# Up-projections of a feed-forward stage as seven products of quarters, on one core

## What is computed

```python
# x: 4608 x 512, w1, w2, w3: 512 x 768, w_out: 768 x 512, all float32
def _moe2_ref(x, w1, w2, w3, w_out):
    h = np.maximum(np.maximum(x @ w1, x @ w2), x @ w3)
    return (h @ w_out).astype(np.float32)
```

## Time and profile before

| | |
|---|---|
| median of 3 runs | 1120.35 us (1119.95 to 1121.66) |
| the profiled execution | 1120.02 us, its span 1118.2 us |
| mean granted clock of TensorE | 0.998 of full speed |
| first and second stage | 0 to 523.52 us |
| third stage | 523.52 to the end, nine blocks |
| bytes moved by DMA | 90.83 MB, mean 81 GB/s |

### The profile page before, as it was taken

The page is one execution under the profiler, slowest core; times in us unless marked ns, Lnnn a source line. Parts: engine busy times, 40 slices in busy tenths (PEclk is TensorE's granted clock), DMA queues, the critical chain, the costliest instruction groups (busy, mean ns, idle before and its releaser), DMA issues.

```text
span 1118.2 us, 14218 instructions
## 1 busy us (share of the span) xinstructions
PE 1099.5 (98%) x5938; PEld 890.4 (80%) x5938; DVE 464.0 (41%) x798; ACT 339.1 (30%) x555; POOL 144.9 (13%) x133
## 2 busy tenths in 40 slices
PE   7999999999999999999999999999999999999998
PEld 5776676888888888888888888888888888888887
DVE  3775677786568476551221302122131212212121
ACT  5566665334334324321121211212121121211211
POOL 0011453322033200237000000000000000000000
PEclk9999999999999999999999999999999999999999
DMA  9997852431231221113001020200102010010100
GB/s 261 324 263 234 233 196 105 137 115 39 78 116 57 97 78 38 57 50 127 32 24 52 1 76 1 76 1 20 57 1 76 1 60 16 19 58 1 38 1 38
DMA packets 65198, 90.83 MB, mean 81 GB/s; under 512 B 19696, under 2 KB 44272, under 8 KB 63472
## 3 DMA queue, kind: packets, MB, share of 16 engines
q1 hardware_dynamic: 61648, 73.81, 20.9%
q0 software_dynamic: 3488, 16.13, 4.1%
HBM read 61.21 MB, written 30.80 MB: 82 GB/s over the span
## 4 chain that ended last, share of the span: by engine, by line
PE 95%; ACT 3%; DMA 1%; DVE 1%; issue 0%; SPq 0%; ACTq 0%
PE ps L1033 39%; PE ps L587 27%; PE ps L1041 13%; PE ps L762 3%; PE ps L942 3%; PE ps L807 2%; PE ps L596 2%; PE ps L732 2%; DMA k_raw<-in_k_dram 1%; PE ps L691 1%; ACT packed L1155 1%; PE ps L786 1%; ACT ost L1307 1%; ACT a2T L1079 1%; PE ps L637 0%
## 5 line engine op out<-in xcount | busy, mean ns | idle before, releaser
L1033 PE MATMUL ps<-ys_lo,w_s_hi 128*128 128x512 f32 x648 | 252.1, 389 | 0.0
L1033 PE MATMUL ps<-ys_hi,w_s_hi 128*128 128x512 f32 x648 | 252.1, 389 | 0.0
L1033 PE MATMUL ps<-ys_hi,w_s_lo 128*128 128x512 f32 x648 | 252.1, 389 | 0.0
L1579 DVE TENSOR_TENSOR second<-ps,first 128x512 f32<-128x512 f32 x54 | 37.4, 692 | 305.7 <-PE ps L1033 305.7
L1033 PEld LDWEIGHTS ps<-ys_lo,w_s_hi 128*128 128x128 f32 x648 | 121.6, 188 | 25.3
L1033 PEld LDWEIGHTS ps<-ys_hi,w_s_hi 128*128 128x128 f32 x648 | 121.6, 188 | 25.3
L1033 PEld LDWEIGHTS ps<-ys_hi,w_s_lo 128*128 128x128 f32 x648 | 121.6, 188 | 25.2
L1079 ACT ACTIVATE h_hi<-third 128x512 fp32r<-128x512 f32 x54 | 34.1, 632 | 304.7 <-DVE third L1583 304.7
L587 PE MATMUL ps<-ln_hi,w_out_s_lo 128*128 128x512 f32 x280 | 109.0, 389 | 0.0
L587 PE MATMUL ps<-ln_lo,w_out_s_hi 128*128 128x512 f32 x280 | 108.9, 389 | 0.0
L587 PE MATMUL ps<-ln_hi,w_out_s_hi 128*128 128x512 f32 x280 | 108.9, 389 | 0.0
(11 more groups left out here) (140 smaller groups left out, 1411.4 us busy)
## 6 DMA issues: line engine op xcount, KB each, us to landing
y_features<-yst SPq DMA_DIRECT2D x9, 1024.0 KB, 4.5
y_raw<-y_features SPq DMA_DIRECT2D x9, 1024.0 KB, 5.4
out_dram<-ost SPq DMA_DIRECT2D x36, 256.0 KB, 2.1
k_raw<-in_k_dram SPq DMA_DIRECT2D x32, 256.0 KB, 5.9
v_raw<-in_v_dram SPq DMA_DIRECT2D x8, 1024.0 KB, 6.8
q_raw<-in_q_dram SPq DMA_DIRECT2D x32, 256.0 KB, 5.3
m_merged<-merged POOLq DMA_DIRECT2D x5, 1024.0 KB, 5.1
weight_raw<-in_moe_w_dram POOLq DMA_DIRECT2D x9, 512.0 KB, 4.3
```

The source lines that it names most:

```text
L1033: last = pe.matmul(ps[:, 3 * (c % 2) + w, :], w_max3[w][a][:, kk, c * P:(c + 1) * P], ys[z][:, kk, :], start=(kk == 0 and e == 0), stop=(k ...
L1579: dve.tensor_tensor(tmp2[c % 2][:, :], ps[:, 3 * (c % 2) + 1, :], tmp1[c % 2][:, :], ALU.max)\
```

## The change

For four pairs of blocks (1024 tokens each) the three up-projections are made as seven products of quarters in place of eight (Strassen's scheme in Winograd's form). The weight is cut in halves of its 512 inputs and, for an index i of 0 to 2, in the chunks i and i + 3 of its outputs; y is cut in halves of its features and in its two blocks. A group (`GROUPS` = 9 in a pair) is one i and one of w1, w2, w3. Its seven products go into four banks, three of them on top of what stands there (`PRODUCTS`: weight operand, y operand, bank). ScalarE copies the first product (`copy_first`) and the third (`copy_fifth`), VectorE adds up the quarters of the result, C11 in the bank itself, C21, C22 and C12 in SBUF (`spot` tiles), and keeps the maxima over w1, w2, w3 in four `best` tiles. In the third group of an i, ScalarE's `hi_h2` and VectorE's `low` split the four. The ninth block is computed as before, in groups of two banks (`plain_group`).

The operands of y are seven, three of them copies and four sums (T1 to T4), made by `hi_y` and `lo_y` in two halves of a pair. Those of the weights (S1 to S4 among them) are made and split by GpSimd in the second stage (`split_operands`, nine sets), stored in DRAM (`w_operands`) and streamed back by SyncE, one load of 128 x 3584 values for each group, in a ring of three buffers (`load_slot`). The output projection runs over a pair at once, eight tiles in eight banks. SBUF is laid out anew, and `y_raw` takes half of a pair at a time. Stages one and two are otherwise as before.

```diff
+GROUPS = 3 * MH
+RING = 3
+A21, A22, A11, A12, S1, S2, S3, S4 = range(8)
+B11, B21, B22, T1, T2, T3, T4 = range(7)
+PRODUCTS = ((A11, B11, 0), (S2, T2, 1), (S1, T1, 2), (A22, T4, 3), (A12, B21, 0), (S3, T3, 1), (S4, B22, 2))
...
+    w_dram = nc.dram_tensor("w_operands", (GROUPS, P, 8, 2, KH, P), F32).ap()
...
+            def load_slot(g):
+                t, s = divmod(g, GROUPS)
+                if g >= RING:
...
+                    sp.wait_ge(g_filled, group_end(g - RING))
...
+                    dst, src = slots[g % RING][:, :, :, :, :], w_dram[s][:, 1:8]
...
+                             src.rearrange("p o e k n -> p (o e k n)")).then_inc(slot_loaded[g % RING], 16)
...
+                for s in range(GROUPS):
+                    load_slot(GROUPS * t + s + RING)
+                for j in range(TPF):
+                    store_out(TPF * t + j)
+                    if j == 1 and t < FOUR - 1:
+                        sp.wait_ge(y_split, 2 * Y_PARTS * (t + 1) + Y_PARTS)
+                        load_y(t + 1, 1)
...
+            def split_operands(s):
+                n = W2_END + s
...
+                add(0, 0, raw[:, A21], raw[:, A22], ALU.add, 4 * s)
+                add(1, 2, raw[:, A11], raw[:, A21], ALU.subtract, 0)
+                add(2, 1, sums[:, 0, :, :], raw[:, A11], ALU.subtract, 4 * s + 1)
+                add(3, 3, raw[:, A12], sums[:, 1, :, :], ALU.subtract, 4 * s + 3)
...
+                pool.tensor_scalar(stage[:, 0:4, 0, :, :], raw, 1.0, None, ALU.mult).then_inc(weight_hi, 1)
+                pool.wait_ge(weight_hi, n + 1)
+                pool.tensor_tensor(stage[:, 0:4, 1, :, :], raw, stage[:, 0:4, 0, :, :].bitcast(F32), ALU.subtract)\
+                    .then_inc(weight_split, 1)
+                wait_alone(pool, weight_split, n + 1)
+                pool.dma_start(w_dram[s][:, 0:4], stage[:, 0:4, :, :, :].bitcast(F32)).then_inc(w_stored[0], 16)
...
...
+                pool.tensor_scalar(stage[:, 4:8, 0, :, :], sums[:, :, :, :], 1.0, None, ALU.mult).then_inc(sums_hi, 1)
+                pool.wait_ge(sums_hi, s + 1)
+                pool.tensor_tensor(stage[:, 4:8, 1, :, :], sums[:, :, :, :], stage[:, 4:8, 0, :, :].bitcast(F32),
+                                   ALU.subtract).then_inc(sums_split, 1)
+                pool.wait_ge(sums_split, s + 1)
+                pool.dma_start(w_dram[s][:, 4:8], stage[:, 4:8, :, :, :].bitcast(F32)).then_inc(w_stored[1], 16)
...
             for t in range(1, BLOCKS):
-                if t == BLOCKS - 1:
-                    wait_alone(pool, h_filled, 32)
-                    split_piece(W1_END)
                 block_scale(t)
-                if t < W1_END:
-                    split_piece(t)
-            split_pieces(W1_END + 1, W1_END + 3)
-            wait_alone(pool, h_filled, TPB * BLOCKS)
-            split_pieces(W1_END + 3, len(pieces))
+                for _ in range((0, 1, 2, 1, 1, 2, 1, 1, 0)[t]):
+                    split_operands(s)
+                    s += 1
...
+            def group(g):
...
+                pe.wait_ge(slot_loaded[g % RING], 16 * (g // RING + 1))
...
+                for n, (a, b, k) in enumerate(PRODUCTS):
+                    if n == 4:
+                        pe.wait_ge(first_copied, g + 1)
+                    elif n == 5:
+                        pe.wait_ge(second_ready, g + 1)
+                    elif n == 6:
+                        pe.wait_ge(fifth_copied, g + 1)
+                    if s == 0 and n in (0, 1, 2, 3, 5):
+                        pe.wait_ge(y_split, 2 * Y_PARTS * t + Y_PARTS + (1, 2, 3, 5, 0, 6)[n])
+                    for kk in range(KH):
+                        for e, (i, j) in enumerate(PASSES):
+                            last = pe.matmul(ps[:, group_bank(g, k), :], w[:, a - 1, i, kk, :], ys[:, b, j, kk, :],
+                                             start=n < 4 and kk == 0 and e == 0,
+                                             stop=kk == KH - 1 and e == len(PASSES) - 1, skip_group_check=n >= 4)
+                    last.then_inc(g_filled, 1)
...
+            def outputs(t, tiles):
...
+                down2(TPF * t, early)
+                down2(TPF * t + 1, early)
+                pe.wait_ge(h2_split, base + parts * (MH - 1) + 2)
+                down2(TPF * t, late)
+                down2(TPF * t + 1, late)
...
+            for t in range(FOUR):
+                for s in range(GROUPS):
+                    group(GROUPS * t + s)
+                outputs(t, TPF)
...
+            def hi_y(t, kk):
...
+                copy(ys[:, B11:B21 + 1, 0, kk, :], y_raw[:, :, 0, :]).then_inc(y_hi, 1)
+                act.wait_ge(turn_ready, 4 * half + 2)
+                copy(ys[:, T2, 0, kk, :], turn[1][:, :]).then_inc(y_hi, 1)
+                copy(ys[:, T1, 0, kk, :], turn[0][:, :]).then_inc(y_hi, 1)
+                copy(ys[:, B22, 0, kk, :], y_raw[:, 1, 1, :]).then_inc(y_hi, 1)
+                act.wait_ge(turn_ready, 4 * half + 3)
+                copy(ys[:, T4, 0, kk, :], turn[1][:, :]).then_inc(y_hi, 1)
+                act.wait_ge(turn_ready, 4 * half + 4)
+                copy(ys[:, T3, 0, kk, :], turn[0][:, :]).then_inc(y_hi, 1)
...
+            def copy_first(g):
+                act.wait_ge(g_filled, FILLS * g + 1)
+                if g >= 2:
+                    act.wait_ge(third_ready, g - 1)
+                copy(firsts[g % 2][:, :], ps[:, group_bank(g, 0), :]).then_inc(first_copied, 1)
...
+            def hi_h2(g):
...
+                for ready, m, c in ((best11, 0, 0), (best21, 1, 0), (best22, 1, 1), (best12, 0, 1)):
+                    act.wait_ge(ready, best_count(g))
+                    copy(h2[0][:, MH * m + i, c * BLK:(c + 1) * BLK], best[m][c][:, :]).then_inc(h2_hi, 1)
...
+                    copy_first(g)
+                    copy_fifth(g)
+                    if s % 3 == 0:
+                        copy_best(g)
+                    elif s % 3 == 2:
+                        hi_h2(g)
+                if t < FOUR - 1:
+                    hi_y(t + 1, 0)
+                else:
+                    hi_last_y()
+                for j in range(2):
+                    copy_out(TPF * t + j)
+                if t < FOUR - 1:
+                    hi_y(t + 1, 1)
+                for j in range(2, TPF):
+                    copy_out(TPF * t + j)
...
+            def lo_y(t, kk):
...
+                dve.tensor_tensor(turn[0][:, :], b12, b11, ALU.subtract).then_inc(turn_ready, 1)
+                dve.wait_ge(turn_ready, turns + 1)
+                dve.tensor_tensor(turn[1][:, :], b22, turn[0][:, :], ALU.subtract).then_inc(turn_ready, 1)
+                dve.wait_ge(y_hi, his + 1)
+                lo(ys[:, B11:B21 + 1, 1, kk, :], y_raw[:, :, 0, :], ys[:, B11:B21 + 1, 0, kk, :]).then_inc(y_split, 1)
...
+                low(4, B22, b22)
+                dve.wait_ge(y_split, his + 2)
+                dve.tensor_tensor(turn[1][:, :], turn[1][:, :], b21, ALU.subtract).then_inc(turn_ready, 1)
+                dve.wait_ge(y_split, his + 3)
+                dve.tensor_tensor(turn[0][:, :], b22, b12, ALU.subtract).then_inc(turn_ready, 1)
+                dve.wait_ge(turn_ready, turns + 4)
+                low(5, T4, turn[1][:, :])
+                low(6, T3, turn[0][:, :])
...
+            def group(g):
...
+                dve.wait_ge(first_copied, g + 1)
+                dve.wait_ge(g_filled, FILLS * g + 2)
+                wait(dve, c12_ready, g)
+                add(second_sum, bank[1], firsts[g % 2][:, :], second_ready)
+                if w > 0:
...
+                    keep(0, 0, bank[0], best11)
+                dve.wait_ge(g_filled, FILLS * g + 6)
+                wait(dve, c22_ready, g)
+                add(third_sum, bank[1], firsts[g % 2][:, :], third_ready)
+                dve.wait_ge(third_ready, g + 1)
+                dve.wait_ge(fifth_copied, g + 1)
...
+                c21, c22, c12 = (part[0], part[1], part[0]) if w else (best[1][0], best[1][1], best[0][1])
+                add(c21, third_sum[:, :], bank[3], c21_ready, ALU.subtract)
+                add(c22, third_sum[:, :], fifths[g % 2][:, :], c22_ready)
+                if w == 2:
...
+                    low(1, 0, 0)
+                if w > 0:
+                    dve.wait_ge(c21_ready, g + 1)
+                    if w == 2:
+                        dve.wait_ge(best21, best_count(g) - 1)
+                    keep(1, 0, c21[:, :], best21)
+                    dve.wait_ge(c22_ready, g + 1)
+                    if w == 2:
+                        dve.wait_ge(best22, best_count(g) - 1)
+                    keep(1, 1, c22[:, :], best22)
+                dve.wait_ge(second_ready, g + 1)
+                dve.wait_ge(g_filled, FILLS * g + 7)
+                if w > 0:
+                    dve.wait_ge(best21, best_count(g))
+                add(c12, bank[2], second_sum[:, :], c12_ready)
+                if w == 2:
+                    low(2, 1, 0)
+                if w > 0:
+                    dve.wait_ge(c12_ready, g + 1)
```

(6 more changed lines are left out.)

535 lines of the change are left out of this document (347 added, 188 removed).

## The result

The changed kernel takes **1072.55 us** (median of 4 runs, 1071.46 to 1072.93). The kernel before took 1121.01 us beside it (4 runs, 1119.95 to 1123.04). The ratio is 0.9564, 95% interval 0.9548 to 0.9581, so the change saves 4.4%, or 48.5 us. The forecast was 1073.0 us. The profiled execution after has a span of 1071.0 us against 1118.2: 47.2 us less.

A forecast was written before the change was run, and what follows sets the result against it. TensorE, busy for 98% of the span, was taken as the limit. 1120.0 - 49.0 - 3.5 + 4.0 + 1.3 = 1072.8 us, with 0.3 for the median 1073 us; range 1067 to 1090 us.

The forecast's parts named there:

- Removed matmuls: Third stage: four pairs of blocks save 216 up-projection matmuls at 0.2267 us each, -49.0 us.
- Output tiles' wait: Output projection: with a bank per tile, the third tile's 0.39 us wait for ScalarE's copy goes nine times, -3.5 us.
- nine blocks are alike: Third stage of the old kernel: each of nine blocks was taken to have the same 0.39 us idle.
- Boundaries: After third groups inside a pair TensorE waits for ScalarE's copy, 0.5 us at 8 boundaries: +4 us, bounds 0 to 16.
- GpSimd in the second stage: GpSimd's added work makes VectorE wait at shared SBUF interfaces, tightest in block 1: +1.3 us, bounds 0 and 5.6.
- rival 3: Second stage: GpSimd stalls VectorE throughout, at the reloads' splits, some 12 us more, 1085 us; chance 0.07.
- Operand stream: Loads of 1792 KB of weight operands per group keep pace with the groups, so TensorE doesn't wait: 0 us.
- Rival 4: The weight operand stream becomes the bound at 13.7 us per load: 62 us more, 1135 us; chance 0.05.
- Operands of the next pair: ScalarE and VectorE make the next pair's y operands during the output matmuls, with 4 us of slack: cost 0.
- Start of the third stage: The first pair's operands are ready in time with 3 us of cover, cost 0; start within 2 us of 523.5.
- Rival 1: VectorE's bunch of 13 operations is longer, 2 us per boundary: 1085 us, up to 1090; chance 0.20.
- rival 2: No wait at the boundaries, ScalarE's chain being 0.4 us shorter, and block 1 hides its delay: 1068 us; chance 0.08.

The follow-up runs named there:

- e2: Changed kernel with ScalarE's copy of the next group's first product moved ahead of the last conversion of a set: 1068.38 us, ratio 0.9531.
- e7: Changed kernel with the fourth product of each group taken over half its inputs, 108 matmuls left out: 1051.89 us, ratio 0.9382.
- e4: Kernel before the change, with only the third output tile moved to bank 0: 1117.87 us beside 1120.83, ratio 0.9971.
- e1: The changed kernel measured once more, nothing altered: 1071.59 us, ratio 0.9562.
- e8: Changed kernel with GpSimd's second and third split of the output projection's weights moved behind its products of block 1: 1071.51 us, ratio 0.9559.
- e9: Changed kernel with both ScalarE's copy moved ahead and GpSimd's two output-weight splits moved later: 1068.97 us, ratio 0.9537.
- e5: Changed kernel with an unused DRAM-to-DRAM copy of 768 KB ahead of each slot load of a pair: 1071.54 us, ratio 0.9554.
- e6: Changed kernel with an unused DRAM-to-DRAM copy of 1792 KB ahead of each slot load of a pair: 1078.56 us, ratio 0.9621.
- e3: Changed kernel with one more, unused 128x512 VectorE maximum ahead of the maximum of C22 in each third group: 1077.26 us, ratio 0.9610.

## Why the prediction was right

- **Removed matmuls, -49.0 us: exact.** 378 matmuls take 85.68 us where nothing waits (e2), 0.22667 each. e7 shows that a matmul less is worth this only as long as no boundary is near.
- **Output tiles' wait, -3.5 us: the mechanism is right and the size was 4.0 (e4).** The step that was off is "nine blocks are alike": 0.39 us was read from the first block, and the eight blocks to 1049.32 us take 65.73 us on average, not 65.67.
- **Boundaries, +4 us: 2.9 to 3.2 measured (e1, after; removed in e2).** Place and releaser are right. Two errors in the step nearly cancel. The bunch ran 0.3 us earlier than I had it: the copy ends at 559.95, which is 5.46 us into the fourth group against the 5.79 of the prediction. The first operation starts 0.04 us behind the product, not 0.26. But TensorE needs the copy earlier than at the fifth product's slot, since the first weight load of that product runs ahead of it (next section), and I took 0.1 us for picking up again. From 560.00 to 588.96 lie 126 matmuls, 28.56 us, and it took 28.96. I had read 8.45 us for 36 matmuls in the earlier trace rows and put 0.16 us of the surplus down to latency; all 0.29 us of it was lost.
- **GpSimd in the second stage, +1.3 us: 0.5 measured (table, e8, e9).** The meeting was at the place named, the split of A in block 1, but VectorE waited 0.8 us there and TensorE lost 0.4. I had taken 1.3 between bounds of 0 and 5.6, and the upper bound counted the whole 2.79 us of GpSimd's split as the wait, while VectorE was held for the first third of such an operation only (last section). Longer waits came in blocks 6 and 7 (a split of A took 3.55 us) and cost TensorE nothing. The blocks named in rival 3 were right but for block 3, where GpSimd was done with its splits at 309.18, ahead of VectorE's at 309.55.
- **Operand stream, 0: right,** 7.3 us to landing and no wait. e5 and e6 put a size to the reserve: copies of 768 KB beside each load of 1792 KB are free, and copies of 1792 KB cost 6 to 7 us, nearly all in the first pair. **Rival 4's threshold was worked out wrongly.** It took the time to landing as the time a load holds the queue (9.52 + 6R). In e6 loads took about 14 us to land, over both its thresholds (11.1 and 13.1), and kept step with the groups after the start, though the time to landing there includes the copy ahead.
- **Operands of the next pair, 0: right.** The second half was issued 13.4 us after the outputs began (625.82 - 612.42) and worked off at 26.5 us; predicted were 14.6 and 27.
- **Start of the third stage within 2 us of 523.5: missed,** 525.93. No operand was late; 1.9 of the 2.4 us are the first stage's scatter, which no term of the sum held.

By these sizes the sum of the third stage is -48.96 - 4.0 + 3.2 = -49.8, against -49.6 measured. Adding +0.5 and +1.9 gives -47.4, against -47.2. That the forecast of 1073.0 came within 0.5 us of 1072.55 is in part luck: its three small terms together were 2.1 us too high (0.5, 0.8 and 0.8), and in the profiled execution the first stage made up 1.9 of that. The second measurement, e1, gave 1071.59. Rival 1 would have shown as boundaries of 2 us, rival 2 as none, and rival 3 as a second stage 12 us longer. The rows show eight boundaries of 0.40 us and a second stage 0.5 us longer.

## What to carry to other kernels

Where an engine that is the limit loses work, look at what it was covering. Here each of 36 groups gave up a seventh product, and the waits sit only where the helpers' operations bunch. There is no slack there, so an operation added is paid for in full (e3), and the matmuls saved between the bunch and the release it holds back save nothing (e7). When an in-order engine releases the limiting one, look at what stands ahead of that release in its queue: moving one copy by one place was worth 3.2 us. Count the release as due at the weight load, not at the matmul: here that was some 0.4 us earlier, and made a cost of what looked like a tie.

## What the runs showed of the hardware

- **The release of a matmul stream is due at its weight load.** TensorE's weight loads around the first boundary of the changed kernel:

```profile
555.01 4.50 PEld L1168 LDWEIGHTS ps<-ys,slot 128*128 128x128 f32 x20
560.00 5.13 PEld L1168 LDWEIGHTS ps<-ys,slot 128*128 128x128 f32 x23 [0.49 <-ACT spot L1243]
```

  The 150 matmuls ahead end their slots at 525.93 + 34.00 = 559.93, so the copy that ended at 559.95 looks on time. But the weight load of the fifth product had been held for 0.49 us by then, and 0.40 us were lost. Four kernels fall in one line, the weight load's mean wait against the mean loss of a boundary or block: after 0.49 and 0.40, before 0.58 and 0.45, e3 1.09 and 0.97, e7 1.16 and 1.04 us (the losses of e3 and e7 from 87.62 us for 378 matmuls and 81.65 for 351); e1, the changed kernel again, gives 0.49 and 0.36. The loss is the weight load's wait less about 0.1 us. No kernel here had a mean wait between 0 and 0.49 us, so that a wait of 0.1 would cost nothing is only what the line suggests.
- **TensorE's clock in the first stage differs between executions of the same code.** From 20 to 40 us its share was 1.00, 0.91 or 0.83; in all profiles but e5's it drops to half (1.2 of 2.4 GHz) for some microseconds between 28 and 38 us. These are the changed kernel's stretches from 25 to 40 us (columns as in e6); in the first TensorE is busy for 3.27 of 5 us, in the next the clock share is 0.52:

```profile
25.00:30.00 5.00, 3.27 (x43) 2.11 (x44) 3.53 (x9) 2.43 (x6) 0.00 (x0) 1.00 1.09 293
30.00:35.00 5.00, 5.00 (x27) 5.00 (x27) 1.40 (x3) 1.46 (x3) 0.00 (x0) 0.52 1.08 328
35.00:40.00 5.00, 5.00 (x44) 4.76 (x44) 3.08 (x6) 2.22 (x6) 1.04 (x1) 0.80 1.06 375
```

  What decides it stays open. The end of the first stage doesn't follow from it alone: e5 at 1.00 ended at 205.64 and e2 at 0.91 at 205.15.
- **VectorE waits for GpSimd by what GpSimd runs.** VectorE's and GpSimd's timelines of the changed kernel in block 6:

```profile
397.93 3.05 DVE L1578 TENSOR_TENSOR m_even<-m_even 128x2048 fp32r<-128x2048 f32 x1
400.90 3.55 DVE L1578 TENSOR_TENSOR a_even<-a_even 128x1152 fp32r<-128x1152 f32 x1
...
397.76 2.81 POOL L619 TENSOR_SCALAR stage<-sums 128x1024 fp32r<-128x1024 f32 x1
400.65 2.58 POOL L621 TENSOR_TENSOR stage<-sums,stage 128x1024 fp32r<-128x1024 f32 x1
```

  The same two operations take VectorE 2.24 to 2.28 and 1.35 us where GpSimd runs nothing beside them. Beside the TENSOR_SCALAR VectorE took 0.8 us more, as if it had begun about 1 us after GpSimd did (397.76) and not at GpSimd's end (400.57). Block 7 (434.18, 2.45 us beside a start at 433.42) and the kernel before (508.34, 2.26 us beside a start at 508.99) give 0.9 to 1.0 us as well. Beside the TENSOR_TENSOR it took 2.20 us more, as if it had begun at 403.10, close to GpSimd's end at 403.23. The meeting of block 1 is of the first kind, so its 0.8 us are less than a third of GpSimd's operation. This is read from the rows of the traces; no run was made to test it.
- **The time to landing of a DMA is longer than its turn on the queue**: a copy and a slot load of 1792 KB each were issued every 9.5 us, 4.8 us for each, and the loads took 14 us to land, at 350 to 430 GB/s (e6).
